# Feed-forward of an attention and experts kernel: the first product of the second half of the tokens by seven products of half matrices

## What is computed

```python
def _moe2_ref(x, w_in, w_out):          # x: 1792 x 768, w_in: 768 x 2048, w_out: 2048 x 768
    h = x @ w_in
    g = np.maximum(0.01 * h, h)
    return (g @ w_out).astype(np.float32)
```

## Time and profile before

| | us |
|---|---|
| median of 3 runs (lowest, highest) | 1220.02 (1219.58, 1221.22) |
| time of the profiled execution | 1221.02 |
| its span | 1219.3 |

### The profile page before, as it was taken

How to read it: one execution, slowest core, us unless ns; L and a number is a source line. 1 busy time by engine, 2 the same in 40 slices (tenths; PEclk the granted TensorE clock), 3 DMA queues, 4 the chain that set the end, 5 groups by cost and what they waited for, 6 DMA issues and landing times. The chain is left out here.

```text
span 1219.3 us, 21715 instructions
## 1 busy us (share of the span) xinstructions
PE 1202.1 (99%) x7301; PEld 1085.9 (89%) x7301; DVE 886.6 (73%) x1138; ACT 744.4 (61%) x1387; POOL 570.7 (47%) x629
## 2 busy tenths in 40 slices
PE   9999999999999999999999999999999999999997
PEld 7888888888889989989989998999999999999997
DVE  6999999999799999999999984555532245552232
ACT  6999999999658788788778773333332222222222
POOL 7998888888226766776776743221010010000010
PEclk9999999999999999999999999999999999999999
DMA  2244334321143555554454144343543421113353
GB/s 74 81 122 120 103 107 105 86 74 47 32 132 136 181 184 183 186 222 161 170 214 157 40 143 118 105 110 99 173 136 119 117 91 53 53 52 104 91 168 104
DMA packets 101756, 144.78 MB, mean 119 GB/s; under 512 B 32136, under 2 KB 72840, under 8 KB 101648
## 3 DMA queue, kind: packets, MB, share of 16 engines
q1 hardware_dynamic: 95888, 115.72, 30.7%
q0 software_dynamic: 5600, 27.68, 7.0%
q10 hardware_dynamic: 160, 0.00, 0.0%
HBM read 205.83 MB, written 19.34 MB: 185 GB/s over the span
## 5 line engine op out<-in xcount | busy, mean ns | idle before, releaser
L983 ACT CAST w_hi<-w_raw 128x768 fp32r<-128x768 f32 (+1 forms) x294 | 249.7, 930 | 21.1 <-DMA w_raw<-moe_w_in 13.6
L1198 DVE TENSOR_TENSOR w_lo<-w_raw,w_hi 128x1024 fp32r<-128x1024 f32 x85 | 183.9, 2198 | 1.3 <-ACT w_hi L983 1.1
L804 POOL TENSOR_TENSOR w_lo<-w_raw,w_hi 128x1024 fp32r<-128x1024 f32 x41 | 102.9, 2513 | 96.3 <-ACT w_hi L983 96.2
L1206 DVE TENSOR_TENSOR w_lo<-w_raw,w_hi 128x768 fp32r<-128x768 f32 x127 | 136.4, 1135 | 0.0
L1584 ACT ACTIVATE small_h<-ps_f 128x448 f32<-128x448 f32 x64 | 34.9, 545 | 161.8 <-PE ps_f L1454 161.8
L432 ACT ACTIVATE probs<-ps_s,neg_max 112x448 f32<-112x448 f32 x192 | 123.1, 652 | 0.0
L1672 DVE TENSOR_TENSOR g_sb<-ps_f,small_h 128x448 f32<-128x448 f32 x64 | 40.0, 624 | 110.7 <-ACT small_h L1584 110.7
L501 DVE TENSOR_REDUCE neg_max<-ps_s 112x2 f32<-112x896 f32 x96 | 104.2, 1085 | 20.5 <-PE ps_s L300 20.4
L923 PE MATMUL ps_y<-w_hi,hT_hi 128*128 128x384 f32 x336 | 116.9, 348 | 0.0
L1551 POOL DMA_INDIRECT out_rows<-y_sb,out_index x9 | 9.6, 1065 | 226.0 <-ACT o_sb L1609 176.8
L507 DVE TENSOR_TENSOR pT_lo<-ps_pt,pT_hi 112x448 fp32r<-112x448 f32 x192 | 113.6, 612 | 2.0 <-ACT pT_hi L441 1.8
(11 more groups left out here) (264 smaller groups left out, 3377.5 us busy)
## 6 DMA issues: line engine op xcount, KB each, us to landing
w_raw<-moe_w_in SPq DMA_DIRECT2D x80, 1536.0 KB
out_raw<-moe_w_out_in SPq DMA_DIRECT2D x64, 384.0 KB, 3.1
in_raw<-moe_w_in_in SPq DMA_DIRECT2D x32, 384.0 KB, 4.3
qk_raw<-q_in SPq DMA_DIRECT2D x48, 112.0 KB, 2.1
qk_raw<-k_in SPq DMA_DIRECT2D x48, 112.0 KB, 2.2
v_raw<-v_in SPq DMA_DIRECT2D x48, 112.0 KB, 2.0
x_rows<-x_tok SPq DMA_DIRECT2D x48, 112.0 KB, 2.6
w_raw<-moe_w_in SPq DMA_DIRECT2D x6, 512.0 KB, 4.4
```

The costliest lines, as they stand in the source:

```text
L804: pool.tensor_tensor(w1_lo[:, c, :], w1_raw[:, c, :], w1_hi[:, c, :].bitcast(F32), ALU.subtract).then_inc(s_w1plo, 1)
L983: act.copy(out[:, c, :], raw[:, c, :]).then_inc(s_hi, 1)
L1198: dve.tensor_tensor(w1_lo[:, c, :], w1_raw[:, c, :], w1_hi[:, c, :].bitcast(F32), ALU.subtract).then_inc(s_w1lo, 1)
L1206: dve.tensor_tensor(w2_lo[:, c, :], w2_raw[:, c, :], w2_hi[:, c, :].bitcast(F32), ALU.subtract).then_inc(s_w2lo, 1)
```

## The change

In the second half the first product is done by a scheme of seven products instead of eight. The hidden blocks p and p + 8 form pair p (8 pairs). w_in's two blocks, cut between contraction blocks 0 to 2 and 3 to 5, give four quarter matrices A; the tokens, cut the same way and, in each tile, between tokens 0 to 63 and 64 to 127, give four B. Seven products `seventh(p, i)` of a quarter or a sum of quarters A with the like of B, 3 contraction blocks x 3 matmuls of 448 columns each, are accumulated in four banks a pair, `v`, `q`, `a`, `b`; the pairs alternate between two sets of banks.

- ACT copies a bank aside after products 0, 1, 3 and 5 (`keep`) and casts A's seven operands (`A_high`, four buffers). DVE makes four sums of A per pair (`sum_A`), the low parts (`A_low`), and from banks and copies the four result blocks with the leaky step (`hidden_part`: an addition and a scalar_tensor_tensor). The result is kept whole in float32 (`g_whole`) and cast and split again in every step of groups 2 and 3 (`g_high`, `g_low`).
- The transposed tokens are copied out whole (`y_copy`), four sums are made (`sum_y`), and quarters and sums are split (`y_high`, `y_low`, `y_sums_high`, `y_sums_low`).
- Groups 0 and 1 now have four and three tiles, and `gT_lo` is one tensor for each. The transposes move to group 1, after the steps of `y_steps`. The loads of y move from SP's queue to POOL's, behind the stores of tiles 0 to 3.
- The ring has four buffers, the fourth being `g_sb`; `slot` names each tile's.
- w_in's blocks come by pairs (`load_pair`); odd pairs land in `raw_odd`, in the room of `gT_lo` of group 1.

The diff, cut to what matters:

```diff
-    groups = ((0, 1, 2), (3, 4, 5, 6), (7, 8, 9, 10), (11, 12, 13))
-    pair = (2, 1, 0, 2, 1, 0, 3, 2, 3, 1, 0, 2, 3, 1)
-    hidden_before = {1: G - 2, 2: G - 1, 9: 2 * G - 2, 10: 2 * G - 1}
-    tile_before = {3: 0, 4: 1, 5: 2, 7: 3, 8: 6, 11: 7, 12: 8, 13: 9}
+    K = C // 2
+    L = G // 2
+    M = P // 2
+    groups = ((0, 1, 2, 3), (4, 5, 6), (7, 8, 9, 10), (11, 12, 13))
+    pair = (2, 3, 1, 0, 2, 1, 0, 2, 3, 1, 0, 2, 3, 1)
+    hidden_before = {2: G - 2, 3: G - 1}
+    tile_before = {4: 0, 5: 2, 6: 3, 11: 7, 12: 8, 13: 9}
+    slot = (0, 1, 2, 3, 0, 1, 2, 0, 1, 2, 3, 0, 1, 2)
+    y_steps = {3: 0, 5: 1, 6: 2, 8: 3, 9: 4, 11: 5, 12: 6}
...
+        with nc.sbuf_tensor("g_whole", [P, G, W], F32) as g_whole:
...
+        raw_odd = [whole[:, u * DM:(u + 1) * DM].rearrange("p (c f) -> p c f", c=C) for u in range(2)]
...
+        g_part = [gT_lo[1][:, at:at + 8 * P], gT_lo[0][:, 0:8 * P]]
...
-        ring = [o_sb, y_g[0], y_g[1]]
+        ring = [o_sb, y_g[0], y_g[1], g_sb]
...
+        def sum_bank(p, name):
+            if p % 2 == 1:
+                return ps[:, "vqab".index(name), 0:Q]
+            return {"v": y_banks[:, 0, 0:Q], "q": y_banks[:, 1, 0:Q], "a": ps[:, 4, 0:Q], "b": ps[:, 5, 0:Q]}[name]
...
-            def load_y(j):
-                if j < 2:
-                    sp.wait_ge(s_xss, J)
-                    sp.wait_ge(s_lg, J)
+            def load_pair(p):
+                if p == 0:
+                    sp.wait_ge(s_inlo, G - 1)
+                elif p == 1:
+                    sp.wait_ge(s_used, 2 * G)
                 else:
-                    sp.wait_ge(s_yt, j - 1)
-                sp.dma_start(y_g[j % 2][:, 0:DM], y_rows[(TILES + j) * P:(TILES + j + 1) * P, 0:DM]).then_inc(s_yg[j % 2], 16)
+                    sp.wait_ge(s_inlo, G - 1 + 7 * (p - 1))
+                for u in range(2):
+                    f = p + u * L
...
             for step in range(2 * G):
                 load_out(step, step % 2)
-                if 2 <= step < TILES + 2:
-                    load_y(step - 2)
-            for f in range(G):
-                load_in(G + f, f % 2)
-            for step in range(2 * G, 4 * G):
+                if step == G:
+                    load_pair(0)
+            for p in range(1, L):
+                load_pair(p)
+                if p < 3:
+                    load_out(2 * G + p - 1, (p - 1) % 2)
+            for step in range(2 * G + 2, 4 * G):
                 load_out(step, step % 2)
...
+            def seventh(p, i):
+                n = 7 * p + i
+                if n == 0:
+                    pe.wait_ge(s_yhi, 2 * TILES)
+                    pe.wait_ge(s_ylo, 2 * TILES)
+                    pe.wait_ge(s_yraw, TILES)
+                if i == 0 and p > 1:
+                    pe.wait_ge(s_c, 4 * (p - 1))
+                    pe.wait_ge(s_aside, 2 * G + 4 * (p - 1))
+                for half in range(2):
+                    if (p, i) == (0, 2):
+                        pe.wait_ge(s_copied[half], groups[1][0] + 1)
+                    if (p, i) == (1, 0):
+                        pe.wait_ge(s_copied[half], TILES)
+                if i in (3, 4, 6):
+                    pe.wait_ge(s_aside, 2 * G + 4 * p + {3: 1, 4: 2, 6: 3}[i])
+                pe.wait_ge(s_inhi, G + n)
+                pe.wait_ge(s_inlo, G + n)
+                acc, new = sum_bank(p, "vqavqbv"[i]), i in (0, 1, 2, 5)
+                for c in range(K):
+                    pe.matmul(acc, A_hi[n % 4][:, c, :], B_part[0][i][:, c, :], start=new and c == 0, stop=False, skip_group_check=not new)
+                    pe.matmul(acc, A_lo[n % 4][:, c, :], B_part[0][i][:, c, :], start=False, stop=False, skip_group_check=not new)
+                    last = pe.matmul(acc, A_hi[n % 4][:, c, :], B_part[1][i][:, c, :], start=False, stop=c == K - 1, skip_group_check=not new)
+                last.then_inc(s_h, 1)
...
                 pe.wait_ge(s_outlo, step + 1)
...
+                if g == 0:
+                    pe.wait_ge(s_ghi, f + 1)
+                    pe.wait_ge(s_glo, f + 1)
+                if g > 1:
+                    pe.wait_ge(s_ghi, step - G + 1)
+                    pe.wait_ge(s_glo, step - G + 1)
...
+                        if f == 0 and t == 1:
+                            pe.wait_ge(s_last, 1)
+                        if f == 0 and g == 2:
+                            pe.wait_ge(s_c, 4 * L if t == 10 else 4 * L - 3)
+                            pe.wait_ge(s_aside, 2 * G + 4 * L)
...
-                        if g == 0 and 1 <= f <= TILES:
-                            transpose_y(f - 1)
+                        if g == 1 and f in y_steps:
+                            transpose_y(y_steps[f])
...
+            k = slot[t]
+            if uses(k, t) > 0:
+                engine.wait_ge(s_store[k], 16 * uses(k, t))
+            if t < RING:
+                engine.wait_ge(s_gate, 1)
+            if t == 3:
+                engine.wait_ge(s_glo, G)
+            if t in (5, 6):
                 engine.wait_ge(s_yt, TILES)
-                engine.wait_ge(s_gate, 1)
+            if t == 10:
+                engine.wait_ge(s_g, 2 * G + 4 * L)
...
+                if t == 3:
+                    for j in range(TILES):
+                        load_y(j)
...
+            def y_copy(j):
                 act.wait_ge(s_yt, j + 1)
                 if j == 0:
+                    act.wait_ge(s_store[3], 16)
+                if j > 0:
+                    act.wait_ge(s_ysum, 4 * j)
+                    act.wait_ge(s_yhi, 2 * j - 1)
+                    act.wait_ge(s_ylo, 2 * j - 1)
+                act.copy(y_flat.rearrange("p (b n) -> p b n", b=2), y_banks[:, :, 0:DM // 2]).then_inc(s_yraw, 1)
...
+                act.wait_ge(s_h, 2 * G + 7 * p + i + 1)
+                if p == 0 and i == 0:
+                    act.wait_ge(s_used, 2 * G)
+                if p > 0:
+                    act.wait_ge(s_c, 4 * (p - 1) + (1, 4, 2, 3)[k])
+                act.copy((e1, e5, e6, e4)[k], sum_bank(p, "vq-v-b"[i])).then_inc(s_aside, 1)
...
+                if i in (1, 3, 4, 6):
+                    act.wait_ge(s_S, 4 * p + {1: 1, 3: 2, 4: 3, 6: 4}[i])
+                if n < 4:
+                    act.wait_ge(s_h, 2 * G)
+                else:
+                    act.wait_ge(s_h, 2 * G + n - 3)
+                act.copy(A_hi[n % 4], A_whole(p, i)).then_inc(s_inhi, 1)
...
+                p, k = f % L, len(groups[g])
+                act.wait_ge(s_g, 2 * G + 4 * p + (2 if f < L else 4))
+                if step == 2 * G + 1:
+                    act.wait_ge(s_h, 2 * G + 7 * L)
+                if step > 2 * G + 1:
+                    act.wait_ge(s_used, step - 1)
+                rows = slice((groups[g][0] - TILES) * P, (groups[g][-1] - TILES + 1) * P)
+                act.copy(g_part[step % 2][:, 0:k * P], g_whole[:, f, rows]).then_inc(s_ghi, 1)
...
+                        y = y_steps.get(f - 1) if g == 1 else None
+                        if y is not None:
+                            y_copy(y)
+                            y_high(y)
                         if step < end:
                             out_high(step, step % 2)
+                            if hf == 1:
+                                g_high(step)
+                        if y is not None:
+                            y_sums_high(y)
...
-                        in_high(G, 0)
-                        in_high(G + 1, 1)
+                        for n in range(4):
+                            A_high(n)
...
+                    dve.wait_ge(s_yhi, 2 * j)
+                    dve.wait_ge(s_ylo, 2 * j)
+                B11, B12, B21, B22 = (y_whole[:, k * K:(k + 1) * K, r * M:(r + 1) * M] for k in range(2) for r in range(2))
+                T1, T2, T3, T4 = (y_sums[:, k, :, :] for k in range(4))
+                dve.tensor_tensor(T1, B12, B11, ALU.subtract).then_inc(s_ysum, 1)
+                dve.tensor_tensor(T3, B22, B12, ALU.subtract).then_inc(s_ysum, 1)
+                dve.wait_ge(s_ysum, 4 * j + 1)
+                dve.tensor_tensor(T2, B22, T1, ALU.subtract).then_inc(s_ysum, 1)
+                dve.wait_ge(s_ysum, 4 * j + 3)
+                dve.tensor_tensor(T4, B21, T2, ALU.subtract).then_inc(s_ysum, 1)
...
+                A11, A12, A21, A22 = one[:, 0:K, :], one[:, K:C, :], two[:, 0:K, :], two[:, K:C, :]
+                out, a, b, op = ((S[1], A21, A22, ALU.add), (S[2], S[1], A11, ALU.subtract),
+                                 (S[4], A12, S[2], ALU.subtract), (S[3], A11, A21, ALU.subtract))[k]
+                dve.tensor_tensor(out, a, b, op).then_inc(s_S, 1)
...
+                dve.tensor_tensor(A_lo[n % 4], A_whole(n // 7, n % 7), A_hi[n % 4].bitcast(F32), ALU.subtract).then_inc(s_inlo, 1)
...
+                product, kept, bank, e = ((3, 1, "a", e1), (5, 3, "q", e6), (7, 4, "v", e4), (7, 2, "v", e5))[k]
+                n = 4 * p + k
+                dve.wait_ge(s_h, 2 * G + 7 * p + product)
+                dve.wait_ge(s_aside, 2 * G + 4 * p + kept)
```

(42 more changed lines are left out.)

270 lines of the change are left out of this document (193 added, 77 removed).

## The result

The changed kernel takes 1204.77 us, median of four executions (1203.79 to 1205.88); the kernel before took 1220.41 beside it. Ratio 0.9872, 95% interval 0.9855 to 0.9889: 15.6 us less. The forecast was 1203.4 with a range of 1201.9 to 1208.0, so the time lies 1.4 us above the point. In the gain itself 1.0 us is missing (15.6 for 16.6); the other 0.4 is the kernel before, which took 1220.41 here where the forecast started from 1220.02. The profiled execution took 1205.64 us, span 1203.9.

The account below looks back on a forecast made before the run. PE bound the kernel: matmuls times their spacing, plus three small gaps. The terms -14.6 - 1.0 - 1.7 + 0.2 + 0.5 = -16.6 us, off the median 1220.02, gave 1203.4 us, range 1201.9 to 1208.0.

Parts of the forecast that it names:

- part 1: Product stage: seven products for eight, 72 fewer matmuls at 0.2024 us each; -14.6 us.
- rival 4: Product stage: each reopened bank or wait stalls PE by a bump; +4.5, time 1207.9 us, chance 0.07.
- rival 1: Product stage: SBUF-only instructions cost 1.79 times, DVE binds (over 12.75 us a pair); time 1234 us, chance 0.03.
- Loads and banks: Product stage: in_raw loads and the copies aside of PSUM banks come early enough; 0 us.
- (a): Between steps 0 and 1 of group 0: a fourth tile covers DVE's split; -1.0 us, 0.1 left.
- (b): Tile 10, group 3's second step: a fourth ring buffer removes the wait for tile 7's store; -1.7 us.
- rival 2: Group boundaries: a new late piece fills both gaps, so the boundary gains don't come; 1206.1 us, chance 0.12.
- (c): Transposes of y move from group 0 to group 1, same 42; 0 if their inputs are early.
- (d): End of group 1: the last y's casts and sums, then the first splits, are ready before PE comes; 0.
- rival 5: Start of the second half: a 2 to 4 us wait from y loads or pair 1's transfer; 1206.5 us, chance 0.06.
- Part 4: Groups 2 and 3: splitting g per step adds 0.2 us for late w_out loads and 0.5 before the last step.
- Rival 3: Group 3's 3-tile steps: the split chain doesn't fit, 13 steps x 0.3 = 4 us; 1207.3 us, chance 0.08.

Follow-up runs that it names:

- shortened kernel: The changed kernel with the last of each pair's seven products cut to one of its three contraction blocks, 48 matmuls fewer in all; 1196.88 us.
- mended pair: Changed kernel, last step's splits and group 2's first g split made early: 1201.66 us; kernel before, fourth ring buffer and last w_out split early: 1217.03 us.
- early first split: The changed kernel with g's cast and subtraction for group 2's first step moved ahead, behind products 2 and 3 of the last pair; 1205.41 us.

## Why the prediction held, step by step

- **The bound and the spacing.** Right. 504 matmuls took 101.99 us, 0.2024 each (the 0.189 that the prediction set beside it is 7% too low); 456 in the shortened kernel took 92.2. The mended pair gives 14.60 us for part 1, where the sum has 14.6.
- **No bump for the new waits.** Right: PE is busy 101.99 of 101.99 us, so rival 4 (+4.5) is out.
- **DVE's load.** The prices held. The changed kernel's groups by line and shape (count, busy us, mean ns, idle before) beside the earlier trace rows:

```profile
L1917 DVE SCALAR_TENSOR_TENSOR g_whole<-whole 128x448 f32<-128x448 f32 x16 | 10.0, 625 | 0.5
L1898 DVE TENSOR_TENSOR in_lo<-whole,in_hi 128x384 fp32r<-128x384 f32 x14 | 7.8, 557 | 3.8 <-ACT in_hi L1735 3.6
L1931 DVE TENSOR_TENSOR gT_lo<-g_whole,gT_lo 128x384 fp32r<-128x384 f32 x16 | 8.8, 552 | 0.0
...
L1735 ACT CAST in_hi<-whole 128x384 fp32r<-128x384 f32 x14 | 7.2, 516 | 3.1 <-PE ps_f L1537 3.1
L1720 ACT COPY whole<-ps_f 128x448 f32<-128x448 f32 x20 | 10.7, 534 | 24.0 <-PE ps_f L1537 24.0
```

  The leaky step takes 0.625 us (0.64 taken), a subtraction of 384 columns 0.557 (0.55), the cast 0.516 (0.48). The 1.79 ratio of rival 1 doesn't appear. The Trainium skill, VectorE: DVE Perf Modes, section The TRN2 errata, gives (N + 151)/0.96 ns for an fp32 tensor_tensor; by it an estimate of 557 ns at 384 columns and 624 at 448, and the trace agrees (557, and 617 to 624). DVE is busy 80% of the stage, the lower end of the 80 to 90 named.
- **Rival 1, its point.** The mechanism is real and its point fits: with 13.2 and 16.5 us of DVE's work a pair, the pair takes that work and the 0.43 us of the experiments' own wait (13.66 and 16.94 us), and PE stops in every pair once DVE's lead is used up. So DVE decides over 12.75 us, as the prediction had it; no run lies between 10.1 and 13.2. The kernel with 16.5 us is slower than before, as was said of one over 14.8. From 10.1 us (81.14 over 8 pairs) there are 2.6 us to that point.
- **Loads and banks (0).** Right: no wait of PE for either in the stage.
- **Boundaries of the groups.** (a) Right, -1.02, with 0.05 us of stop left (856.89 + 0.17 to 857.11). (b) Right: -1.71 here and -1.6 where only the buffer was added. So rival 2, in which neither gain comes, is out. (c) and (d) Right, 0: rival 5 doesn't appear.
- **Part 4, late w_out loads (+0.2).** Didn't come. PE has no gap in group 3 up to the last step, and no cast of w_out there waits for a DMA. Rival 3 (+4) is out: the 3-tile chain fits.
- **Part 4, the last step (+0.5).** Right: 1.70 became 2.17 us, +0.47; in the profile's own column 1.54 became 2.01, the 2.0 that was named as a sign.
- **Missed in part 4: the first step of group 2.** The steady steps and the last one were costed, the first was not. Its split stands behind a copy that waits for PE; 0.51 us, which the kernel with the early first split took away.
- **Missed in the sum: the clock behind the last stop.** The sum took a stop at its own length. A 2.17 us stop cost up to 1.62 us more, in some executions. That is the larger part of why the median lies above the point. Between 1203.8 (without) and 1205.8 (with) the median of four is a matter of how many fall on each side: with the fall in all four it would lie 2.4 us above the point, and with none 0.4. How near the point came is in that measure chance; the range holds either.

In sum: -14.1 (with the missed 0.5), -1.0, -1.7, +0.1 in group 2, and +2.3 at the end (0.47 stop, 1.62 clock, 0.2 to 0.3 tail, within the span's rounding) are the -14.45 us of the feed-forward; the forecast's terms gave -16.6. What lacks is the stop before group 2 (0.5) and the end (1.8 more than the 0.5 named), less the 0.2 us of late loads that didn't come. The remaining 0.95 us of the spans lies ahead of the feed-forward, in what the change doesn't touch.

## What to carry to other kernels

On a kernel whose PE has no gaps, a scheme that trades products for sums is worth its matmuls times their spacing, if the engine that makes the sums keeps some room under the new, shorter period. Its load is the sum of the distances from one start to the next, and a wait for its own last instruction counts into it: in an experiment's added line such a wait turned a step of 0.47 us into one of 0.68. When an experiment misses, look at what its own lines wait for before blaming another engine. Then look at the two ends of each stage, not at its middle: the first step, where a new instruction queues behind one that waits for the old stage, and the last, where no work covers the chain. Price a stop of the tensor engine by what comes behind it too: 0.5 us more of stop cost up to 2.1.
